# Even and odd queries as a slot's tiles, inverse sums read in pairs, and an accumulator on three kinds of VectorE instruction

## The reference

```
scores = q @ k.T / sqrt(64)
scores = cap * tanh(scores / cap)
attn   = exp(scores - max(scores))
attn   = attn / (sum(attn) + 1e-09)
x      = attn @ v                      # [2, 12, 448, 64] -> [896, 768]
x = elu(x @ w_in) @ w_out              # 768 -> 2048 -> 768
x = leaky(x @ w_in2) @ w_out2          # leaky: max(0.01 h, h)
```

## Time and profile before

| | |
|---|---|
| median of three runs | 581.84 us (581.84 to 583.5) |
| profiled execution, its own time | 582.32 us |
| its span, first to last instruction | 580.5 us |
| mean granted TensorE clock | 0.997 of full |
| TensorE matmul, busy | 560.0 us (96%) |
| VectorE | 479.3 us (83%) |
| ScalarE | 353.4 us (61%) |
| GpSimd | 281.2 us (48%) |

### The profile page before, as it was taken

One profiled execution on the slowest core, in us unless ns is written; L12 is line 12 of the kernel. 1 busy time (PEld: TensorE's weight loads), 2 busy tenths in 40 slices (PEclk: granted clock), 3 DMA queues, 4 the chain that ended last, 5 costly groups with the idle time before them and its releaser, 6 DMA issues. The chain is left out here.

```text
span 580.5 us, 8583 instructions
## 1 busy us (share of the span) xinstructions
PE 560.0 (96%) x2908; PEld 501.3 (86%) x2908; DVE 479.3 (83%) x731; ACT 353.4 (61%) x606; POOL 281.2 (48%) x273
## 2 busy tenths in 40 slices
PE   7999879999999999999999999989999999999997
PEld 6676758888998999999999999879999998899996
DVE  5899999989887223897999998789999788999871
ACT  5999978999996455654644455445454455544440
POOL 5879998799976656552000002586666520000000
PEclk8999999999999999999999999999999999999999
DMA  6354545445432233335644432031113225536251
GB/s 174 93 150 124 124 127 155 129 123 138 114 86 70 92 110 108 110 108 165 217 137 146 153 85 80 1 109 55 55 55 91 74 82 191 162 111 217 83 169 49
DMA packets 34172, 67.07 MB, mean 116 GB/s; under 512 B 6864, under 2 KB 18768, under 8 KB 34128
## 3 DMA queue, kind: packets, MB, share of 16 engines
q1 hardware_dynamic: 33984, 66.28, 38.9%
q10 hardware_dynamic: 144, 0.23, 0.1%
HBM read 63.70 MB, written 2.80 MB: 115 GB/s over the span
## 5 line engine op out<-in xcount | busy, mean ns | idle before, releaser
L557 POOL TENSOR_TENSOR w_lo<-w_raw,w_hi 128x768 fp32r<-128x768 f32 (+1 forms) x62 | 105.7, 1707 | 55.5 <-ACT w_hi L619 54.9
L557 POOL TENSOR_TENSOR w_lo<-s_sum,w_hi 128x384 fp32r<-128x384 f32 x32 | 37.8, 1195 | 119.1 <-ACT w_hi L619 119.1
L619 ACT ACTIVATE w_hi<-s_sum 128x768 fp32r<-128x768 f32 (+1 forms) x64 | 43.4, 684 | 78.7 <-DVE s_sum L876 54.5
L619 ACT ACTIVATE w_hi<-w_raw 128x768 fp32r<-128x768 f32 (+1 forms) x77 | 56.5, 737 | 31.6 <-PE o_ps L1118 16.0
L599 ACT ACTIVATE soft<-soft,neg_max 112x448 f32<-112x448 f32 x96 | 63.3, 666 | 4.9 <-DVE soft L755 4.8
L755 DVE TENSOR_SCALAR_CACHE_REDUCE soft<-soft,neg_abs 112x448 f32<-112x448 f32 x96 | 60.7, 669 | 2.6 <-ACT soft L589 2.2
L1116 PE MATMUL mlp_ps<-x_hi,w_hi 128*128 128x448 f32 x132 | 49.2, 373 | 0.4 <-issue 0.4
L1117 PE MATMUL mlp_ps<-x_lo,w_hi 128*128 128x448 f32 x132 | 48.2, 365 | 0.0
L1118 PE MATMUL mlp_ps<-x_hi,w_lo 128*128 128x448 f32 x132 | 48.2, 365 | 0.0
L589 ACT ACTIVATE soft<-scores 112x896 f32<-112x896 f32 x47 | 43.1, 918 | 6.8 <-PE scores L1077 6.7
L762 DVE TENSOR_TENSOR p_lo<-probs_t,p_hi 112x896 fp32r<-112x896 f32 x37 | 40.2, 1087 | 6.3 <-ACT p_hi L608 6.2
(11 more groups left out here) (236 smaller groups left out, 1751.5 us busy)
## 6 DMA issues: line engine op xcount, KB each, us to landing
w_raw<-w_units SPq DMA_DIRECT2D x120, 384.0 KB, 3.1
q_raw<-qT SPq DMA_DIRECT2D x24, 224.0 KB, 2.9
k_raw<-kT SPq DMA_DIRECT2D x23, 224.0 KB, 2.8
v_raw<-v_rows SPq DMA_DIRECT2D x24, 112.0 KB, 2.9
inv_all<-inv_rows SPq DMA_DIRECT2D x24, 112.0 KB, 3.1
y_t<-y_out SPq DMA_DIRECT2D x12, 224.0 KB, 2.9
inv_rows<-row_inv SPq DMA_DIRECT2D x24, 1.8 KB, 2.9
k_raw<-kT ACTq DMA_DIRECT2D x1, 224.0 KB, 3.2
```

Of the source, the lines that this page charges most:

```text
L557: pool.tensor_tensor(w_part(w_lo, n), w_source(n), f32(w_part(w_hi, n)), ALU.subtract).then_inc(w_lo_pool, 1)
L619: nc.scalar.activation(w_part(w_hi, n), w_source(n), ACT.Copy).then_inc(w_hi_done, 1)
```

## The change

The queries of a slot are dealt to its two tiles by turns: tile 0 has the even ones, tile 1 the odd ones, instead of the first and the second 112. q is put in that sequence on the host (`by_tile`), so that scores, tanh, maxima and exp stay as they are. The transposes write tile t to every second column of the PSUM bank, starting at t, which restores the queries' sequence; `p_hi`, `p_lo`, the values and O are as before. In the row of inverse sums the two tiles' numbers of a partition now belong to neighbouring queries, so the row is read in pairs: two floats side by side, then two skipped. This holds for VectorE's scaling of heads 0 to 7 and GpSimd's of the others.

The small sum of `invert` and the three roundings of `w_high` on VectorE get another form: a `tensor_scalar` with an accumulator output, whose value goes to a small tensor `unread` that nothing reads. On the chip such a form is two instructions, the operation and the reading of its accumulator.

No instruction changes its place on any engine, no wait is added or removed, and the DMAs keep their sizes.

```diff
+        unread = sb("unread", [P, 2 + AHEAD])
...
-                    rows = x_raw[:, b, :].rearrange("r (t p) -> r t p", t=NQ)
-                    pool.tensor_tensor(rows, rows, inv_all[:, b, :].rearrange("r (p t) -> r t p", t=NQ), ALU.mult
+                    rows = x_raw[:, b, :].rearrange("r (a p t) -> r a p t", a=2, t=2)
+                    pool.tensor_tensor(rows, rows, inv_all[:, b, :].rearrange("r (p a t) -> r a p t", a=2, t=2), ALU.mult
                                        ).then_inc(x_scaled, 1)
...
-                nc.vector.tensor_scalar(row_den[:, h % 2, :], row_sum[:, h % 2, :], EPS, 1.0, ALU.add, ALU.mult
-                                        ).then_inc(den_done, 1)
+                nc.vector.tensor_scalar(row_den[:, h % 2, :], row_sum[:, h % 2, :], EPS, 0.0, ALU.add, ALU.add,
+                                        accum_out=unread[0:QT, h % 2:h % 2 + 1]).then_inc(den_done, 1)
...
-                nc.vector.tensor_tensor(x_raw[rows, m % 2, :].rearrange("r (t p) -> r t p", t=NQ),
-                                        o_bank(h)[0:HD, :].rearrange("r (t p) -> r t p", t=NQ),
-                                        inv_all[0:HD, h % 2, :].rearrange("r (p t) -> r t p", t=NQ), ALU.mult
+                nc.vector.tensor_tensor(x_raw[rows, m % 2, :].rearrange("r (a p t) -> r a p t", a=2, t=2),
+                                        o_bank(h)[0:HD, :].rearrange("r (a p t) -> r a p t", a=2, t=2),
+                                        inv_all[0:HD, h % 2, :].rearrange("r (p a t) -> r a p t", a=2, t=2), ALU.mult
                                         ).then_inc(o_read, 1)
...
-                nc.vector.tensor_copy(w_part(w_hi, n), w_source(n)).then_inc(w_hi_dve, 1)
+                nc.vector.tensor_scalar(w_part(w_hi, n), w_source(n), 1.0, 0.0, ALU.mult, ALU.add, accum_out=unread[:, 2 + n:3 + n]
+                                        ).then_inc(w_hi_dve, 1)
...
-                        col = (c % 2) * 2 * QT + t * QT
-                        last = nc.tensor.transpose(probs_of(k)[0:QT, c // 2, col:col + QT],
+                        col = (c % 2) * 2 * QT + t
+                        last = nc.tensor.transpose(probs_of(k)[0:QT, c // 2, col:col + 2 * QT - 1:2],
                                                    soft[0:QT, k % SOFT, t, c * QT:(c + 1) * QT], ident[:, :])
...
+def by_tile(t):
+
+    return np.ascontiguousarray(t.reshape(NHEAD, P, 2, QT, 2).transpose(0, 1, 2, 4, 3)).reshape(NHEAD, P, SEQ)
...
-        "qT": twice(q),
+        "qT": by_tile(twice(q)),
```

## The result

The changed kernel has a median of 576.8 us (575.49 to 577.57, four runs) against 582.21 for the kernel before on the same chip: a ratio of 0.9901, 95% interval 0.9874 to 0.9927. Two later comparisons on other occasions gave 0.9945 (0.9931 to 0.9959) and 0.9927 (0.9903 to 0.9951), medians 577.4 against 580.74 and 576.75 against 581.18. So the three comparisons put the gain at 0.6 to 1.0%, or 5.4, 3.3 and 4.4 us. The forecast was 578.5 us, faster; its range of 575.8 to 596.0 holds the time.

The account below looks back on a forecast made before the run. TensorE bounds the kernel; other engines can set the time only in the attention up to about 110 us. Terms: 582.3 - 1.8 - 1.5 = 579.0 us profiled, 578.5 beside the median; range 575.8 to 596.

Parts of the forecast that it names:

- The scaling of O, 953 to 620 ns: VectorE's scaling of O (L783), heads 0 to 7: reading floats in twos takes 620 ns, 0.33 us less a head.
- The small sum, 0.24 us always: VectorE's small sum (L770), 24 times: 0.16 us plus 0.08 for the accumulator's extra instruction, against a mean of 0.64.
- A rounding at 1.0 us: VectorE's three weight roundings (L805): 1.0 us each with an accumulator, 0.4 us less at the third, at 71.1 us.
- The transposes at no cost: TensorE's 384 transposes (L1090): writing every second float of the PSUM bank adds 0; bounds up to 47 or 93 ns.
- rivals 1 and 2: Stepped write slows TensorE's transposes: about 594 us (0.20) or more (0.11); VectorE's reading in twos no faster: 580.1 us (0.09).
- How the small sum waits: On VectorE, the small sum queues for something GpSimd holds and would end with the GpSimd instruction each time.
- The five waits for the scaling of O down to 1.2 us: TensorE's five waits for VectorE's scaling of O, 3.0 us in all, shrink to about 1.2 us.
- the 0.65 us: Taken off TensorE's last wait for the scaling of O, 1.02 us, through cheaper VectorE work ahead of it.
- 1.8 us up to 67 us: Up to 67 us, the five TensorE waits for the scaling of O give 1.8 us in all.
- 1.5 us from 67 to 94: Six TensorE waits from 67 to 90 us give 2.0 us, cut to three quarters, 1.5; after 94 us, 0.
- The sum as a sum: Over the whole kernel, the two terms of 1.8 and 1.5 us add up to a gain of 3.3 us.
- Rival 3, ScalarE at once the limit: ScalarE, at 2.89 us a slot, takes over: half of the 3.3 us or less, 580.2 us or above; chance 0.10.

## Why the prediction was right, point by point

*The scaling of O, 953 to 620 ns:* measured 617. *The small sum, 0.24 us always:* 145 ns and 81 ns of reading, never more. *A rounding at 1.0 us:* 0.93. *The transposes at no cost:* 96 ns apart, 259 ns each, and the kernel with contiguous writes takes the same time. So every price of an instruction was right, and rivals 1 and 2 are out. The way was right too, but the size was low: the sum gives 3.3 us, and the profiles are 4.7 us apart and the medians 3.3 to 5.4.

*How the small sum waits:* the prediction says that the rows at 89 us agree with a lock that is held to the end of a GpSimd instruction. They agree only in that the sum ends where a GpSimd instruction ends. That instruction began after the sum, as the timelines under "The roundings alone" show, so the sum did not go by who was there first.

*The five waits for the scaling of O down to 1.2 us:* they are 1.8, from 3.0; two more profiles of the changed kernel have 1.5 and 1.2 in four. In two heads VectorE now waits for the broadcast of the inverse sums, 1.0 us in all:

```profile
41.91 0.62 DVE L785 TENSOR_TENSOR x_raw<-o_ps,inv_all 64x448 f32<-64x448 f32 x1 [0.44 <-DMA inv_all<-inv_rows]
...
54.27 0.62 DVE L785 TENSOR_TENSOR x_raw<-o_ps,inv_all 64x448 f32<-64x448 f32 x1 [0.57 <-DMA inv_all<-inv_rows]
```

I had not asked what would be late next for this instruction. Nor had I asked what else its matmul waits for: the 0.65 us that I took off the last of the five waits was not to be had from VectorE alone, since GpSimd's split of v ended 0.04 us before the scaling of O did. With the pairs alone, three waits for that split came up, 3.0 us in all.

*1.8 us up to 67 us:* the profile has 1.65, of which 0.56 was there before the first scaling of O. That 0.56 comes from the start: in 10 to 15 us the clock before was at 0.66 of full and after at 1.00. It isn't the change's doing: the kernel with contiguous transposes has the low clock there too (0.66), is level with before at slot 6, and is 1.64 us ahead at slot 18 and 4.7 at the end. So what is lost at the start is taken up before slot 18, and this term was about right as a number. The five waits give only 1.2 us of it; where the rest comes from isn't shown.

*1.5 us from 67 to 94:* 3.0. This is the term that was mis-sized, and with it the roundings' share. I had worked out 2.0 and cut a quarter, because ScalarE would be late next. The cut was not needed: ScalarE's own waits for VectorE's maxima in 60 to 110 us fell from 3.6 us in five to this (columns as in the earlier trace rows):

```profile
ACT soft L601 <- DVE soft L757: 0.7, 2, 0.5
```

And I had priced the casts at VectorE's own time, 0.4 us in front of one wait. They also held GpSimd, which hardly rests there: by 2.8 us in twenty in the kernel with the small sum's accumulator only, and by about 2.0 in the kernel before (its four GpSimd instructions around the casts are longer by 0.99, 0.30, 0.45 and 0.31 us). With the other parts made cheaper, GpSimd's split of v is what TensorE waited for. The experiments give 2.0 us for the roundings once the sum is out of the way. The step that failed is "what it removes on VectorE" without "whom it was holding".

*The sum as a sum:* the parts don't add. Roundings alone +5.7 us, small sum alone -1.0, both -3.0 (and -2.5 in the second comparison); pairs alone -0.7, on top of both -1.9. Each part alone leaves a wait that another part removes, and the long waits cost twice, once as the wait and once as some 3 us at the lower clock behind it (6 us behind the longest). The prediction has no term for the clock; the changed kernel didn't need one, since it has 1.00 there. In the kernel before, the casts kept GpSimd late, and so the small sum at 48.21 us met only the end of a short instruction (0.41 us), where with the roundings alone it met a chain of GpSimd work (3.38). That it did so by luck is my reading of the two timelines; it isn't tested.

*Rival 3, ScalarE at once the limit:* partly true. It is at 54.3 of 55 us in the first stretch. A slot takes (65.28 - 28.56) / 12 = 3.06 us on average, near the 3.0 forecast and not the 2.9 of ScalarE's pace. A nearly full ScalarE would also explain why taking the small sum away altogether gives nothing more; no run separates this from the noise.

What stays open: why the three comparisons of the changed kernel lie between 0.9901 and 0.9945, so that the first interval doesn't meet the second (its medians differ by 0.65 us and those of the kernel before by 1.5), and by what order VectorE and GpSimd take turns.

## What to carry to other kernels

Keep a tiny VectorE instruction that GpSimd can hold up off the critical path: look at the longest of its executions against the shortest, not at its mean, and try a form that isn't held. When two engines hold each other up, price both directions. Don't judge such a repair by one half alone: here one half made the kernel 1% slower and both halves 0.4 to 0.6% faster. Before you take a wait off, look at what ends just before its releaser: here the next one stood 0.04 us behind, and a wait grown to 1.8 us halved the granted clock behind it. If an operand must be read with a step, give it a layout in which two neighbours are used from each 16 bytes, and put the step on a writer that has clocks to spare.

## What the runs showed of the hardware

- A single-source VectorE instruction on four floats a partition in SBUF waited 3.2 us behind GpSimd instructions that follow each other without a gap; the form with an accumulator output never waited (136 to 150 ns in 24). The Trainium skill ("SBUF — State Buffer", section "Who interferes with whom") has the lock and names this form as the one without it, and the runs agree. It says that who starts first gets the shared pair; here the one that stood ready was passed over by GpSimd's next instructions, three in the worst case.
- A cast of 128 x 768 took 0.55 us where it was free and up to 1.50 where it wasn't, against 0.93 for the accumulator form. With the small sum's accumulator in place, this form, slower than the free cast, made the kernel 2.0 us faster; without it, 5.7 us slower.
- After TensorE had waited 1.79, 1.93 and 3.99 us (pairs alone, small sum's accumulator alone, roundings alone), its granted clock fell to 0.50 of full, for some 3, 3 and 6 us. With both accumulators, in the changed kernel, and with the roundings alone but without the small sum, no wait of TensorE in 20 to 75 us is longer than 0.8 us, and the clock stays at 1.00. The wait of 2.77 us in the last of the three was not followed by a lower clock.
- TensorE's write to every second float of PSUM: 187 against 96 ns for 224 bfloat16 columns, 96 against 96 ns for a 112 x 112 float32 transpose, and the same with a step of four.
- VectorE's read of 448 floats beside a PSUM operand: 616 ns with steps of 1 and 2 and in pairs out of four or eight, 928 ns with a step of 4. GpSimd: 1128 to 1142 ns against 1352.
